# Who issues the loads of an output weight: from ScalarE's queue to SyncE's

## The reference

```python
# attention: B,H,S,D = 4,8,768,64; chunks of 32 queries see 8 memory keys and the keys
# from 16 before the chunk to 8 behind it
scores = scale * (q_c @ k_full.T); a = softmax(scores); out[:, :, chunk] = a @ v_full
x = attn_out.transpose(0, 2, 1, 3).reshape(3072, 512)
# block A: d_ff = 1536
x = (sigmoid(x @ w_gate) * (x @ w_val)) @ moe_w_out
# block B: d_ff = 2048
h = x @ w_in
g = (a[0] + a[1]*h + a[2]*h**2 + a[3]*h**3) / (1 + abs(b[0])*abs(h) + abs(b[1])*h**2 + 1e-6)
return g @ moe2_w_out
```

## Time and profile before

| | us |
|---|---|
| median of 3 executions | 1212.2 |
| lowest, highest | 1210.92, 1216.8 |
| the profiled execution, its own time | 1210.92 |
| its span (first to last instruction) | 1208.6 |
| PE busy in the span | 1183.2 |
| DVE, ACT, POOL busy | 900.6, 752.9, 119.0 |

### The profile page before, as it was taken

How to read it: one execution, slowest core, us unless ns; L and a number is a source line. 1 busy time by engine, 2 the same in 40 slices (tenths; PEclk the granted TensorE clock), 3 DMA queues, 4 the chain that set the end, 5 groups by cost and what they waited for, 6 DMA issues and landing times.

```text
span 1208.6 us, 21376 instructions
## 1 busy us (share of the span) xinstructions
PE 1183.2 (98%) x8304; PEld 975.2 (81%) x8304; DVE 900.6 (75%) x1393; ACT 752.9 (62%) x1230; POOL 119.0 (10%) x150
## 2 busy tenths in 40 slices
PE   9989999989999998999999999999999999999998
PEld 8978888767888876788888888888888888888887
DVE  3577656656666565667657899998998998988987
ACT  2455555435555544555555787777877877877875
POOL 2113232020232301023200000000000000000000
PEclk9999999989999999999999999999999999999999
DMA  8412421651332255233216500200200200200000
GB/s 283 142 36 78 141 71 60 230 182 48 105 114 95 71 194 194 88 107 112 70 36 238 189 1 1 70 1 1 70 0 0 69 0 0 69 0 0 36 1 35
DMA packets 40721, 97.81 MB, mean 81 GB/s; under 512 B 4288, under 2 KB 4288, under 8 KB 40640
## 3 DMA queue, kind: packets, MB, share of 16 engines
q1 hardware_dynamic: 30272, 77.81, 18.8%
q10 hardware_dynamic: 10368, 18.88, 5.2%
HBM read 84.09 MB, written 12.58 MB: 80 GB/s over the span
## 4 chain that ended last, share of the span: by engine, by line
PE 91%; DVE 4%; ACT 3%; issue 1%; DMA 0%; ACTq 0%; SPq 0%; DVEq 0%
PE ps_h L1107 9%; PE ps_h L1114 9%; PE ps_h L1109 9%; PE ps_h L1214 7%; PE ps_h L1213 7%; PE ps_h L1218 7%; PE ps_y L1251 7%; PE ps_y L1253 7%; PE ps_y L1257 7%; PE ps_y L1152 4%; PE ps_y L1157 4%; PE ps_y L1153 4%; PE ps_y L1077 2%; PE ps_h L1057 2%; PE ps_h L1044 1%
## 5 line engine op out<-in xcount | busy, mean ns | idle before, releaser
L1107 PE MATMUL ps_h<-xop,wop 128*128 128x512 f32 x504 | 198.1, 393 | 7.1 <-ACT probs L428 5.7
L1109 PE MATMUL ps_h<-xop,wop 128*128 128x512 f32 x504 | 196.8, 390 | 0.0
L1114 PE MATMUL ps_h<-xop,wop 128*128 128x512 f32 x504 | 156.4, 391 | 0.0
L1213 PE MATMUL ps_h<-x_split,weights 128*128 128x512 f32 x384 | 149.4, 389 | 0.0
L1214 PE MATMUL ps_h<-x_split,weights 128*128 128x512 f32 x384 | 149.4, 389 | 0.0
L1251 PE MATMUL ps_y<-weights,hid 128*128 128x512 f32 x360 | 140.0, 389 | 0.0
L1253 PE MATMUL ps_y<-weights,hid 128*128 128x512 f32 x360 | 140.0, 389 | 0.0
L743 DVE TENSOR_TENSOR wop<-rawp,wop 128x448 fp32r<-128x448 f32 x144 | 89.6, 653 | 49.3 <-ACT wop L407 49.1
L1107 PEld LDWEIGHTS ps_h<-xop,wop 128*128 128x128 f32 x504 | 95.0, 189 | 30.4 <-ACT probs L428 7.0
L764 DVE TENSOR_TENSOR x_raw<-ps_h,probs_t 128x512 f32<-128x512 f32 x72 | 49.5, 688 | 89.1 <-PE ps_h L1114 88.6
L637 ACT ACTIVATE tmp<-ps_h 128x512 f32<-128x512 f32 x96 | 57.1, 595 | 92.6 <-PE ps_h L1218 92.6
(11 more groups left out here) (90 smaller groups left out, 2281.8 us busy)
## 6 DMA issues: line engine op xcount, KB each, us to landing
oraw<-wo_l ACTq DMA_DIRECT2D x72, 256.0 KB, 2.7
rawp<-wgv_l SPq DMA_DIRECT2D x36, 512.0 KB, 3.3
unit<-v_l SPq DMA_DIRECT2D x24, 520.0 KB, 5.9
unit<-k_l SPq DMA_DIRECT2D x24, 512.0 KB, 5.1
unit<-q_l SPq DMA_DIRECT2D x24, 256.0 KB, 3.7
x_stage<-y_dram SPq DMA_DIRECT2D x6, 1024.0 KB, 5.7
out<-stage SPq DMA_DIRECT2D x24, 256.0 KB, 2.1
braw<-wb_l SPq DMA_DIRECT2D x11, 512.0 KB, 5.8
```

The costliest lines, as they stand in the source:

```text
L1107: nc.tensor.matmul(dst, w_h[k], xop[:, m, 0, k, :], start=first and k == 0, stop=False, skip_group_check=True)
L1109: nc.tensor.matmul(dst, w_l[k], xop[:, m, 0, k, :], start=False, stop=False, skip_group_check=True)
L1114: last = nc.tensor.matmul(dst, w_h[k], xop[:, m, 1, k, :], start=False, stop=k == 1, skip_group_check=True)
L1213: nc.tensor.matmul(dst, lhs(c, 0), x_split[:, 0, c, :], start=(c == 0), stop=False)
```

## The change

`load_oraw` moves from ScalarE's program to SyncE's. The waits (on `wo_lo`), the buffers and the number of transfers stay; what is new is which engine waits and issues, and where in its list the load stands. The coordinates `n + 4` and so on keep the loads two pieces ahead of the copy, or further.

```diff
@@ sync
+            def load_oraw(n):
+                if n >= PIECES:
+                    return
+                wait(sp, wo_lo, n - ORING + 1)
+                sp.dma_start(oraw[:, n % ORING, :], wo[n % TA]).then_inc(oraw_loaded[n % ORING], 16)
...
             sp.dma_start(b_raw, coef_b).then_inc(coef_loaded, 16)
+            load_oraw(0)
+            load_oraw(1)
 
             for s in range(NS):
                 for i in range(NQ):
                     c, n = CHAINS * s + 2 * i, first_piece(s, i)
                     load_raw(c + 2)
+                    load_oraw(n + 4)
...
                     load_raw(c + 3)
+                    load_oraw(n + 5)
...
                 n, g = piece_of(s, 0, TA - 2), UNITS * (s + 1)
+                load_oraw(n + 4)
                 load_qk(g + 2)
+                load_oraw(n + 5)
                 load_qk(g + 3)
+                load_oraw(n + 6)
                 load_v(g + 2)
                 for m in range(4):
                     store_a(2 * s, m)
                 load_v(g + 3)
+                load_oraw(n + 7)
                 for p in (1, 2):
                     load_qk(g + 2 * p + 2)
                     load_qk(g + 2 * p + 3)
+                    load_oraw(n + 2 * p + 6)
                     load_v(g + 2 * p + 2)
+                    load_oraw(n + 2 * p + 7)
                     load_v(g + 2 * p + 3)
+                for ahead in range(12, 16):
+                    load_oraw(n + ahead)
 
             n = piece_of(NS - 1, 0, TA - 2)
             load_braw(B_EARLY)
+            load_oraw(n + 4)
             load_braw(B_EARLY + 1)
+            load_oraw(n + 5)
...
             load_braw(B_EARLY + 2)
+            load_oraw(n + 6)
             for m in range(4):
                 store_a(NT - 2, m)
-            for o in range(B_EARLY + 3, TB - 1):
-                load_braw(o)
+            for ahead in range(7, TA + 2):
+                load_braw(B_EARLY + ahead - 4)
+                load_oraw(n + ahead)
             load_braw(TB - 1)
@@ scalar
-            def load_oraw(n):
...
             def split_wout(n):
-                load_oraw(n + 2)
                 act.wait_ge(oraw_loaded[n % ORING], 16 * (n // ORING + 1))
...
-            load_oraw(0)
-            load_oraw(1)
             attention(0, at_start)
```

## The result

The changed kernel is slower: a median of 1222.9 us (17 runs) against 1212.3 us of the kernel before on the same chip, a ratio of 1.0080 with an interval of 1.0058 to 1.0101. Run again on another chip (five runs) it gave 1220.3 against 1212.6, ratio 1.0060 (1.0036 to 1.0084). One more execution of the changed kernel took 1468.1 us at a granted clock of 0.753; the ratio leaves it out, as a slow one. The profiled execution took 1226.8 us, its span is 1224.7, 16.1 more than before's 1208.6; the second profile's span is 1220.2. The medians lie only 10.6 us apart (7.7 on the second chip), so the first profile shows more than the typical loss.

What follows compares the result with a forecast made beforehand. TensorE, busy throughout the chains, was taken as the bound, leaving gains only in attention phases, first start and beginning. -3.5 - 0.9 + 1.2 = -3.2 us from 1210.9 gave 1207.7, a median of 1209.0, range 1205 to 1213.

Steps and rivals of the forecast that it cites:

- Part 1: Attention phases, pairs p = 1, 2, 3: without the load between ScalarE's two copies, exponents come 1.20 us sooner; -3.5 us.
- what is late next: Attention phases, p = 1: once 1.20 us is won, TensorE's next wait is still the exponent, by 0.13 us.
- the stall of 1.88 us: Second superstep's attention: a TensorE wait with no releaser before the p = 2 turn, taken to cover the gain there: 0.
- Part 2: The beginning: the first two oraw loads go behind the first phase's last v, so first scores come sooner; -0.9 us.
- Part 3, v of the sixth unit: Attention phase: v goes out behind piece n+6, about 464.1; 1.1 us to spare to 1.6 late, taken as 0.
- the same bounds: Attention phase: q and k behind that v are needed some 2 us later, again 1.1 us to spare to 1.6 late.
- rival C: The stream blocks: v lands in its median time, clock falls, snapshot waits grow; +7.0 us, median 1219, chance 0.14.
- Part 3, the weights of the third chain: End of attention phases: the late load puts GpSimd's sums beside VectorE's T4 work; 0.6 us in each of two supersteps, +1.2.
- Part 4: Last fourteen pieces: oraw loads share one stream with other tiles and stores; lateness up to 1.6 us, taken as 0.
- Block B: Block B is not touched by the change: 0.
- D: It doesn't do what it says: something else holds ScalarE's second copy; 0 to -1 us, median 1212, chance 0.12.

Runs made afterwards that it cites:

- the spread: TensorE's two back-to-back groups of 64 small matmuls get a third of a piece between them: kernel before 1212.5 us, copy_first 1210.6, order_last_act 1210.6.
- copy_first: The kernel before, with ScalarE's load of piece n+2 moved behind its copy of piece n, all loads staying on ScalarE: 1214.2 us, ratio 1.0007.
- order_last_act: event_order, with the ten loads issued during the last fourteen pieces back on ScalarE: 1211.4 us, ratio 1.0001.
- raw_first: The changed kernel, with the third chain's weights issued ahead of the attention phase's last four oraw loads: 1217.65 us, ratio 1.0044.
- tiny_sums: The changed kernel, with GpSimd's third-chain sums in supersteps two and three cut to one column in 256: 1215.5 us, ratio 1.0038.
- waits_only: The kernel before, with SyncE making the changed kernel's waits in its attention list while ScalarE keeps the loads: 1218.0 us, ratio 1.0056.
- event_order: The changed kernel, all loads on SyncE, each attention list written in the order in which its waits are fulfilled: 1212.9 us, ratio 1.0003.

## Why the prediction was wrong

*Part 1, -3.5 us.* The mechanism is right and the worth of it wrong. ScalarE's two copies of a pair stand back to back, and the exponents' waits of p = 1 and 2 are gone in both supersteps:

```profile
449.22 1.14 ACT L436 ACTIVATE wout<-oraw 128x512 fp32r<-128x512 f32 x2
```

The step that failed is "what is late next". I looked for it among the engines, and took the stall of 1.88 us as a thing of one place. TensorE's supply of instructions was next, by the timing of its packets and by what the spread does: copy_first turned 2.47 us of waits into 2.77 of stalls and 0.47 of a piece's wait.

*Part 2, -0.9.* The wait for the first k is gone, and the scores start at 6.10 us instead of 6.59, not before 5.8 as forecast, since TensorE's own warm-up now ends there (in order_last_act it starts at 5.4). The first chain comes 1.2 us sooner, 66.3 against 67.5. Right in size.

*Part 3, v of the sixth unit, 0.* This is the step that failed first: the loads in the burst were given their least landing, and so no cost. Its issue was forecast for 464.1 and came at 463.83; I then took the least landing, 3.2 us, where the median was 5.9, and it took 6.0; TensorE went on at 469.95. TensorE waited 1.22 us, as rival C had it. In the second profile this v landed after 4.4 us and nobody waited for it; there the k issued at 462.42, which I had put at "the same bounds", took 6.4 us, and TensorE waited 1.69. The bound was wrong for the whole burst: eight loads issued within 4.6 us, 3.1 MB, need nearly 10 us at the 322 GB/s measured there (an estimate), and the last v of it takes 8.2. Behind it stand stalls of 3.57 and 1.84 us. That the burst makes them is not shown: raw_first, tiny_sums and waits_only have the burst and no stall there. The clock fell at this place too: 0.90 over the 70.9 us of this phase in the second profile (some 7 us). event_order, which takes the block away, has no wait for q, k or v left.

*Part 3, the weights of the third chain, +1.2.* Right in kind, and too small beyond its own bound: both pairs are slowed, by 1.8 us in the third superstep instead of 0.6 (bound 1.1), in the second a third pair too, and the snapshot waits are 3.67 and 3.97 us instead of 2.4, so 1.9 and 2.1 more than before. The bound came from one pair of L735 in the first superstep; L731 beside GpSimd takes 2.34. The rule of the Trainium skill that was set beside it ("GPSIMD Engine Reference", section 1, Specifications) said that both would be slowed: the traces bear it out, and even its 1 us more was too little. With what the clock adds, this term is 7 us by waits_only, 3 to 5 by the ratios of tiny_sums and 2 to 4 by those of raw_first, against the 1.2 of the sum; I had given the clock no term in the likeliest case.

*Part 4, 0 (0 to 1.6).* In the last pieces ScalarE waits for an `oraw`, and TensorE behind it; first ScalarE, then TensorE, changed kernel:

```profile
671.95 0.63 ACT L436 ACTIVATE wout<-oraw 128x512 fp32r<-128x512 f32 x1 [3.10 <-DMA oraw<-wo_l]
677.92 0.63 ACT L436 ACTIVATE wout<-oraw 128x512 fp32r<-128x512 f32 x1 [3.35 <-DMA oraw<-wo_l]
```

```profile
679.33 0.50 PE L1165 MATMUL ps_y<-hid,wout 128*128 128x512 f32 x1 [1.28 <-DVE wout L761]
```

With a second one of 0.25 that is 1.5 us, and 0.24 + 0.23 in the second profile: within the bounds. But waits_only, which moves no load there, has 0.31 + 0.27, so the moved loads are not all of it.

*Block B, 0.* Right, to 0.1 us.

*The rivals.* C is what happened: forecast 1219, measured 1222.9 and 1220.3, by its mechanism in the main (loads that land in their median time, the snapshots, the clock behind them). That it is near is partly luck: it kept 2.4 us of part 1, which came back as stalls, and put 2.2 on the snapshots, which cost 4.1 without the clock. I held its condition, a landing of over 4.3 us, for the less likely side although the median landing on record was 5.9. D has its rule (the Trainium skill, "DMA: Bandwidth & Descriptors", section "Issuing engines are not separate DMA queues") half borne out: the issuer as such makes no difference that can be measured (event_order, 1.0003), but which waits stand ahead of a load in its issuer's list makes 0.6 to 0.8%.

*The sum.* The 16.1 us between the profiled spans, by kind. TensorE's idle time: -0.5 in the second superstep's attention (5.80 us of waits of 0.4 and more against 6.27), +1.9 for its snapshot, +6.1 in the third's attention (11.6 against 5.5), +2.1 for its snapshot, +1.5 in the last pieces: 11.1. The lower clock, half of each stretch in which it was granted: 10.2 us against 5.1, +5.1. The start: -1.2. Together 15.0; 1.1 us are left without a name. The forecast had -3.5, -0.9 and +1.2 in the first kind and the start, and nothing for the clock.

## What to carry to other kernels

Moving a load to another engine moves its wait too: write down for each entry behind it in the new list when it went and when it can go now, with the median landing and not the least. A helper whose work ran in a quiet stretch (here GpSimd) may come to run beside an engine on which others wait (here VectorE) once a late load shifts it, and slow it. And when a wait of the busiest engine goes, ask whether its own instruction supply is next; here it helped to put long instructions between two dense groups of small ones.

## What the runs showed of the hardware

- TensorE stalls 0.4 to 3.6 us, mostly in the middle of 64 small matmuls (0.8 us for the group), until 1.0 to 1.6 us after a 16 KB packet of the instruction queue has ended. With two such groups back to back 20 of the 22 phases profiled show one to four such stalls; with a third of a piece between them one kernel of three had one, the two others none.
- VectorE's pairs with two operands in SBUF, 1.28 us alone, take 1.8 to 2.35 us beside GpSimd's; GpSimd's own sum of 0.74 mostly takes 1.06 to 1.19.
- Of eight loads of 256 to 520 KB issued within 4.6 us, the v and k (second to last) took 6.0 to 8.2 us to land in one profile and 4.4 to 8.3 in the other.
- An idle time of TensorE costs more than itself: behind the snapshot waits of 3.88 and 3.97 us the granted clock was at its lower level for 6.8 us, behind those of 3.54 to 3.67 for 3.4 or not at all, behind those of 1.75 to 2.15 in the second and third supersteps not at all in 15 of 22 cases and for 3.4 us in 7. The changed kernel around its last snapshot: 0.84 over 22 us, 3.5 us, nearly the wait once more; around the stall of 3.57 it was 0.68 over 16 us.

```profile
476.00:492.00 16.00, 12.93 (x184) 10.03 (x185) 6.32 (x11) 4.26 (x8) 0.00 (x0) 0.68 0.20 68
500.00:522.00 22.00, 17.95 (x65) 13.88 (x65) 16.56 (x27) 10.64 (x19) 6.63 (x8) 0.84 0.36 120
```

- 64 semaphore increments at the start of TensorE's stream moved its first product from 1.53 to 10.57 us, at least 0.14 us for each (the 1.53 were spent waiting for GpSimd, and may hide some).
